# Half of w_in's remainders through ScalarE and an adding DMA, the convolution's steps dealt out anew, narrow banks added straight from PSUM

## What is computed

```
x:   4 x 4096 x 192,  weight_gen: 4 x 4096 x 8 heads x 7 taps
w    = softmax(weight_gen over the 7 taps)          (with + 1e-9 in the divisor)
conv[b,s,h,:] = sum_k w[b,s,h,k] * x[b, s-6+k, head h's 24 channels]
h    = conv @ w_in          (16384 x 192) @ (192 x 2048)
g    = h * sigmoid(1.702 h)
out  = g @ w_out            (16384 x 2048) @ (2048 x 192)
```

## Time and profile before

| | us |
|---|---|
| runs shown | 1143.32, 1144.75, 1146.94 |
| median | 1144.75 |
| the profiled execution's own time | 1144.86 |
| its span in the profile | 1143.0 |
| TensorE busy / weight loads | 1117.3 / 919.4 |
| VectorE busy | 811.0 |
| ScalarE busy | 618.5 |
| GpSimd busy | 6.5 |
| DMA | 41.89 MB, 37 GB/s on average |

### The profile page before, as it was taken

How to read it: one execution, slowest core, us unless ns; L and a number is a source line. 1 busy time by engine, 2 the same in 40 slices (tenths; PEclk the granted TensorE clock), 3 DMA queues, 4 the chain that set the end, 5 groups by cost and what they waited for, 6 DMA issues and landing times.

```text
span 1143.0 us, 21688 instructions
## 1 busy us (share of the span) xinstructions
PE 1117.3 (98%) x9748; PEld 919.4 (80%) x9748; DVE 811.0 (71%) x719; ACT 618.5 (54%) x652; POOL 6.5 (1%) x8
## 2 busy tenths in 40 slices
PE   6999979999999999999999999999999999999998
PEld 4787768888888888888888888888888888888886
DVE  7888698859587594876849578595876949678322
ACT  6466646554555645556455464645555455544543
POOL 2000000000000000000000000000000000000000
PEclk9999999999999999999999999999999999999999
DMA  7600110100101001010110101001010010100000
GB/s 243 206 15 15 52 34 20 39 29 1 39 29 39 29 1 65 2 39 29 35 33 1 39 28 40 29 1 57 11 38 29 13 55 1 39 29 1 29 1 29
DMA packets 8492, 41.89 MB, mean 37 GB/s; under 512 B 1040, under 2 KB 1296, under 8 KB 6096
## 3 DMA queue, kind: packets, MB, share of 16 engines
q1 hardware_dynamic: 8400, 40.51, 10.7%
HBM read 24.77 MB, written 12.58 MB: 33 GB/s over the span
## 4 chain that ended last, share of the span: by engine, by line
PE 91%; DVE 6%; ACT 2%; issue 1%; DMA 0%; ACTq 0%; DVEq 0%; SPq 0%
PE hid L593 43%; PE acc_main L609 28%; PE acc_rest L609 19%; DVE prod L362 1%; DVE conv L369 1%; DVE gate_lo L513 1%; ACT gate_hi L302 1%; DMA gate<-in_x_first 0%; ACT gate L299 0%; ACT xt L256 0%; DVE hid L443 0%; DVE w L415 0%; DVE xt L395 0%; DVE prod L387 0%; DVE prod L437 0%
## 5 line engine op out<-in xcount | busy, mean ns | idle before, releaser
L299 ACT ACTIVATE gate<-hid 128x1024 f32<-128x1024 f32 x256 | 263.0, 1028 | 479.6 <-PE hid L593 478.9
L513 DVE TENSOR_TENSOR gate_lo<-gate,gate_hi 128x1024 fp32r<-128x1024 f32 x256 | 312.4, 1220 | 252.2 <-ACT gate_hi L302 251.4
L593 PE MATMUL hid<-xt,w_hi 64*128 64x512 f32 x3072 | 433.6, 388 | 5.9 <-ACT xt L256 4.3
L593 PEld LDWEIGHTS hid<-xt,w_hi 64*128 64x128 f32 x3072 | 289.3, 185 | 68.6 <-issue 6.6
L609 PE MATMUL acc_main<-gate_hi,w 64*128 64x512 f32 x2048 | 317.1, 388 | 5.9 <-DVE gate_lo L513 5.9
L302 ACT ACTIVATE gate_hi<-hid 128x1024 fp32r<-128x1024 f32 x256 | 261.1, 1020 | 0.0
L609 PEld LDWEIGHTS acc_main<-gate_hi,w 64*128 64x128 f32 x2048 | 192.2, 185 | 47.5 <-DVE gate_lo L513 7.6
L593 PE MATMUL hid<-xt,w_lo 64*128 64x512 f32 x1536 | 216.8, 387 | 0.0
L609 PE MATMUL acc_main<-gate_lo,w 64*128 64x512 f32 x1024 | 200.2, 387 | 0.0
L609 PE MATMUL acc_rest<-gate_hi,w 64*128 64x512 f32 x1024 | 200.0, 387 | 0.0
L609 PE MATMUL acc_rest<-gate_lo,w 64*128 64x512 f32 x1024 | 199.9, 387 | 0.0
(11 more groups left out here) (51 smaller groups left out, 225.0 us busy)
## 6 DMA issues: line engine op xcount, KB each, us to landing
xwin<-in_x_runs SPq DMA_DIRECT2D x15, 1056.0 KB, 4.9
out<-outs_main SPq DMA_DIRECT2D x13, 512.0 KB, 2.6
out<-outs_rest SPq DMA_DIRECT2D x13, 256.0 KB, 2.9
taps<-in_tap_runs SPq DMA_DIRECT2D x1, 3136.0 KB, 10.2
taps<-in_w_rows SPq DMA_DIRECT2D x2, 1536.0 KB, 9.8
w_hi<-w_hi SPq DMA_DIRECT2D x2, 768.0 KB, 9.0
w_lo<-w_lo SPq DMA_DIRECT2D x2, 768.0 KB, 7.2
out<-outs_main SPq DMA_DIRECT2D x6, 256.0 KB, 2.0
```

The costliest lines, as they stand in the source:

```text
L299: nc.scalar.activation(gate[:, v % 2, :, :], hid[:, v % 2, :, :], ACT.Gelu_apprx_sigmoid).then_inc(gate_ready, 1)
L513: nc.vector.tensor_tensor(gate_lo[:, v % SLOTS, :, :], gate[:, v % 2, :, :], gate_hi[:, v % SLOTS, :, :], ALU.subtract).then_inc(gate_lo_r ...
L593: last = nc.tensor.matmul(hid[:, v % 2, h, :], w[rows, k if j else slice_of(h, k), q, f], xt[rows, j % 2, part, k, :], start=(i == 0), sto ...
```

## The change

Three things are changed.

1. **Remainders of w_in, columns 512 to 1,023.** VectorE's two instructions for them go. ScalarE writes -w_hi of these columns into `w_lo` (behind w_hi at the start), GpSimd issues a DMA that adds it onto `w_raw` in place (128 x 1,536 elements), and ScalarE rounds the sum into `w_lo` in two parts at n = 2 and n = 4. The rounding of w_out on ScalarE is cut in three: two parts before unit 0, the third behind unit 0.
2. **Order of the steps.** STEPS_AT has new numbers, and the steps now come from a list (STREAM) in which the four softmax steps of the piece after stand ahead of the split of the piece before. Rounding moves to v = 5 in pieces 1 and 2, and the crossings have units of their own (CROSS_HI_AT, CROSS_LO_AT). For piece 1 VectorE takes over one of the two remainder crossings.
3. **Emptying a narrow main bank.** VectorE no longer copies it into SBUF; it adds it straight from PSUM onto what ScalarE lifted, in two halves, before the `rest` half.

```diff
-STEPS_AT = ((0, 4, 2, 3, 2, 3, 3, 2),
-            (2, 2, 3, 3, 3, 3, 3, 3),
-            (1, 2, 3, 2, 3, 5, 1, 2),
-            (1, 1, 2, 2, 2, 2, 2, 4),
-            (0, 0, 0, 5, 2, 1, 2, 1, 2, 2, 1, 2, 0, 1, 0, 0))
-ROUND_AT = (7, 7, 7, 7, 12)
+STEPS_AT = ((0, 6, 2, 4, 2, 2, 2, 3),
+            (3, 3, 5, 1, 4, 5, 2, 2),
+            (0, 3, 3, 4, 2, 5, 0, 3),
+            (1, 1, 1, 1, 3, 3, 0, 4),
+            (0, 0, 1, 2, 4, 1, 2, 0, 0, 0, 3, 3, 2, 0, 1, 0))
+ROUND_AT = (7, 5, 5, 7, 12)
+CROSS_HI_AT, CROSS_LO_AT = (7, 6, 5), (7, 7, 5)
...
-            sp.wait_ge(w1_lo_ready, 5)
+            sp.wait_ge(w1_lo_ready, 3)
+            sp.wait_ge(w1_late_ready, 2)
             sp.dma_start(w1_lo[LOWER, :, 1, :].bitcast(F32), w1_lo[UPPER, :, 0, :].bitcast(F32)).then_inc(w1_doubled, 16)
...
                 act.wait_ge(xt_lo_ready, j)
-                for there, here in ((LOWER, UPPER), (UPPER, LOWER)):
+                for there, here in ((LOWER, UPPER), (UPPER, LOWER))[0:1 if j == 1 else 2]:
...
             nc.scalar.activation(w1_hi[:, :, 0, :], w1_raw, ACT.Copy).then_inc(w1_hi_ready, 1)
-            act.wait_ge(w2_loaded, 16)
-            nc.scalar.activation(w2_of(0, 2, slice(0, D)), w2_of(0, 2, slice(0, D), w2_raw), ACT.Copy
-                                 ).then_inc(w2_hi_ready, 1)
+
+            act.wait_ge(w1_hi_ready, 1)
+            nc.scalar.activation(w1_lo[:, :, 0, LATE], w1_hi[:, :, 0, LATE].bitcast(F32), ACT.Copy, scale=-1.0
+                                 ).then_inc(w1_negated, 1)
...
-            nc.scalar.activation(w2_of(2, CH // 2, slice(0, D)), w2_of(2, CH // 2, slice(0, D), w2_raw), ACT.Copy
-                                 ).then_inc(w2_hi_ready, 1)
+            act.wait_ge(w2_loaded, 16)
+            for at in (0, 2):
+                round_w2(at, at + 2)
...
+                    if n == 0:
+                        round_w2(4, CH // 2)
                     if n == 1:
                         exponentials(1)
                         exponentials(2)
+                    if n in (2, 4):
+                        at = slice((n + 2) * P, (n + 4) * P)
+                        act.wait_ge(w1_added, 16)
+                        nc.scalar.activation(w1_lo[:, :, 0, at], w1_raw[:, :, at], ACT.Copy).then_inc(w1_late_ready, 1)
...
-                        if is_narrow(j + 1):
+                    if is_narrow(j) and is_narrow(j + 1):
+                        if v == CROSS_HI_AT[j]:
                             cross_rounded(j + 1)
+                        if v == CROSS_LO_AT[j]:
                             cross_remainders(j + 1)
...
+        STREAM = [(1, q) for q in range(STEPS)] + [(2, q) for q in range(STEPS - 1)]
+        for j in range(3, LAST + 1):
+            STREAM += [(j, q) for q in range(SOFTMAX_STEPS)] + [(j - 1, STEPS - 1)]
+            STREAM += [(j, q) for q in range(SOFTMAX_STEPS, STEPS - 1)]
+        STREAM += [(LAST, STEPS - 1)]
...
+                if j == 1:
+                    dve.wait_ge(xt_lo_ready, 1)
+                    nc.vector.tensor_copy(other(j, UPPER, 1), own(j, 1)[LOWER].bitcast(F32)).then_inc(lo_crossed, 1)
...
+            def evict_main(j):
                 dve.wait_ge(main_added, UNIT0[j + 1])
+                if is_narrow(j):
+                    dve.wait_ge(main_out_act, j + 1)
+                    for to, done in ((FORE, main_summed), (AFT, main_out_dve)):
+                        of = to if j == 0 else AFT if to == FORE else FORE
+                        nc.vector.tensor_tensor(outs_main[:, 0, to], acc_main[:, 1, of], outs_main[:, 0, to], ALU.add
+                                                ).then_inc(done, 1)
+                else:
+                    wait(dve, main_stored, 16 * j)
+                    nc.vector.tensor_copy(outs_main[:, 1, :], acc_main[:, 1, :]).then_inc(main_out_dve, 1)
...
-                    if j == 0 and v in (1, 3):
-                        w1_remainder(slice((v + 3) * P, (v + 5) * P))
...
+            pool.wait_ge(w1_negated, 1)
+            pool.dma_start(w1_raw[:, :, LATE], w1_lo[:, :, 0, LATE].bitcast(F32), accum_op=ALU.add).then_inc(w1_added, 16)
...
-                    if n in (0, 1, 2, 4, 6) and i == SLICES:
-                        pe.wait_ge(w1_lo_ready, n + 1 if n < 2 else n // 2 + 2)
+                    if n in (0, 1, 2) and i == SLICES:
+                        pe.wait_ge(w1_lo_ready, n + 1)
+                    if n in (4, 6) and i == SLICES:
+                        pe.wait_ge(w1_late_ready, n // 2 - 1)
```

34 lines of the change are left out of this document (17 added, 17 removed).

## The result

| | before | after |
|---|---|---|
| median of the runs, us | 1144.79 (4 runs, 1143.32 to 1146.94) | **1128.98** (4 runs, 1128.95 to 1129.13) |
| ratio, 95% interval | | **0.9861** [0.9844, 0.9878] |
| span of the profiled execution | 1143.0 | 1127.2 |

The forecast was 1130.2, in a range of 1127.5 to 1137.5; the change is 1.2 us better than that. The kernel before scatters by more than this, and the interval of the ratio stands for a gain of 14.0 to 17.9 us, so the terms are compared in the traces, not in these times.

What follows compares the result with a forecast made beforehand. TensorE, busy for 98% of the span, was taken as the bound. Losses at the start and four piece changes fall from 19.6 to 4.9 us, so 14.7 are won: 1144.86 - 14.7 = 1130.2 us, range 1127.5 to 1137.5.

Steps and rivals of the forecast that it cites:

- Start: First units: the loss goes from 1.0 to 1.3 us, with ScalarE's added rounding and negation nearly free.
- The adding DMA: GpSimd's DMA onto w_raw at the start: lands at 26.8 us, needed at 29.1, so it costs 0.
- rival A: At the start: the adding DMA is late, landing at 33.3, costing 3.4 us and giving 1133.6; chance 0.09.
- Change 0 to 1: From piece 0 to 1: the loss falls from 4.2 to 1.3 us, 0.75 of it waiting for gate_lo(7).
- Change 1 to 2: From piece 1 to 2: the loss falls from 1.0 to 0.3 us, with gate_lo(7) due when ready.
- Change 2 to 3: From piece 2 to 3: the loss falls from 4.9 to 1.15 us, with gate_lo 0.3 and 0.5 late.
- Change 3 to 4: From piece 3 to 4: the loss falls from 8.5 to 0.85 us, with gate_lo(6) 0.5 late.
- Adding from PSUM: Narrow pieces: a copy of 0.69 us goes, the adds wait 0.6 for ScalarE's lift, so 0 is won.
- Wide pieces: Wide pieces: nothing lost; gate_lo(5) starts 6.6 us after gate(5), done at 7.8, wanted at 8.6, 0.8 in reserve.
- rival C: Wide pieces: gate_lo(5) over 0.8 us late costs each of 13 pieces; 1158.8 with the burst 3 us longer; chance 0.04.
- Rival B: Last two changes: count off by a microsecond or two, stalls over 2.5 us plus half clock, 1137; chance 0.13.
- Rival D: Whole kernel: TensorE's waits pass to another, such as the lift behind the crossings; 1144; chance 0.04.

Runs made afterwards that it cites:

- e5: Kernel after, with GpSimd waiting for gate_hi of unit 1, so the adding DMA is issued at 25.0 us: 1132.02 us.
- e6: Kernel after, with GpSimd waiting for gate_hi of unit 2, so the adding DMA is issued at 29.5 us: 1137.83 us.
- e8: Kernel after, with one step of piece 3's row moved behind the turn and no three first products in a row from piece 2 to 3: 1128.32 us.
- e9: Kernel after, with the crossings left at v = 7 at every change: 1137.03 us.
- e10: Kernel after, with the last steps of piece 4, the turn among them, moved behind the last gate_lo of piece 3: 1131.06 us.
- e2: Kernel after without the third part: the narrow main bank is copied into SBUF and added there: 1129.69 us.
- e7: Kernel after, with five wide steps in place of four in the burst at v = 4 of the wide pieces: 1144.51 us.
- e3: First and third parts alone: kernel after with the old order of steps, rounding and crossings: 1145.21 us, ratio 1.0005 to before.

## Why the prediction was right, point by point

**What bounds the kernel.** Held. Wide pieces are still 68.91 us long, 16 x 4.307, and all that was won is from the ledger.

**Start, 1.3.** Was 1.05, and TensorE has no wait there, where I had counted 0.1 and 0.2. Gate of unit 2 came at 27.15 (27.2 forecast) and the first rounding of w_lo ended at 29.8 (30.0).

**The adding DMA, 0.** Held in the kernel as it is: landing 27.5 for 26.8. It was right about the queue (engines full until w_hi's pair is through) and nearly about its work. I halved 9.0 us because the bytes are half of the pair's, which says that an adding DMA runs as fast as a copy: its bytes do move at 191 to 195 GB/s for a copy's 215 to 225. What the halving left out are the 2 us before the first bytes, which e5 and e6 show and which in the kernel after passed behind the pair. What failed is that I let each late microsecond cost one: 2.10 us of waiting cost 3.95, by the clock. So rival A's landing at 33.3 would have cost more than the 3.4 us that I gave it: e5, landed at 32.0, is 3.0 above the kernel after, where by my rule it pays 2.1. The wait that rival A rests on did not come. GpSimd's issue takes 1.42 us in the kernel after, in e5 and in e6, and in e6 the bytes move from 31.5 on, while VectorE's timeline has no gap between 28.98 and 32.88 (gate_lo, remainders of w_out, a multiplication and an addition). The Trainium skill ("SBUF — State Buffer", on SBUF's two sides) has a GpSimd DMA held behind VectorE's 2-port operations; its widest reading, that any work of VectorE holds the DMA back, falls by these rows, and its narrow one was not tried, as no float32 copy ran there. The estimate of 3.8 us worked out from the Trainium skill ("DMA: Bandwidth & Descriptors", on the anatomy of a DMA from GpSimd) does not hold for this transfer: 6.6 us is the least that was measured. Its fixed 2.0 us are near what e5 and e6 show, its 436 GB/s are not.

**Change 0 to 1, 1.3.** Was 1.04: gate_lo(7) at 48.33 for 48.8, TensorE's recorded wait 0.39 for 0.75. It costs more than is recorded: the weight loads idle 0.81 in front of it, and e5 and e6, which do not have it, are 0.68 shorter there. So 0.68 stands against 0.75 and the other 0.37 against the 0.3 that I added to each change: here the working was right.

**Change 1 to 2, 0.3.** Was 0.37, and a cause for it, which I had taken from the ledger as it stood, can now be read. Three first products stand in a row, and the third writes the `hid` that ScalarE still reads for the first. The row of 12 matmuls at 90.19 takes 1.81 where the one at 88.15 takes 1.52, and the weight loads of L630 wait 0.42 for gate_hi at 91.03, and the same 0.42 at each of the other three changes. That this is the 0.37 was not tried by itself: at the change 2 to 3, e8 does without the three in a row, and a wait of 0.44 for another buffer comes in its place.

**Change 2 to 3, 1.15: the term that was mis-sized.** Was 0.41. I had gate_lo(6) late by 0.3 and the first one of piece 3 by 0.5. VectorE's timeline at units 5 and 6, and the weight load that wants gate_lo(6):

```profile
108.72 1.22 DVE L548 TENSOR_TENSOR gate_lo<-gate,gate_hi 128x1024 fp32r<-128x1024 f32 x1
...
115.68 1.22 DVE L548 TENSOR_TENSOR gate_lo<-gate,gate_hi 128x1024 fp32r<-128x1024 f32 x1 [0.41 <-ACT gate_hi L313]
...
116.96 0.30 PEld L646 LDWEIGHTS acc_main<-gate_hi,w 64*128 64x128 f32 x4 [0.18 <-DVE gate_lo L548]
```

Gate of unit 5 starts at 106.37, so VectorE comes to gate_lo(5) 2.35 behind it and not 2.8. The steps behind that took about what I gave them, the split ends 5.57 behind gate(5) for 6.15, and gate_lo(6) 10.53 for 11.1; it is wanted at 10.6 to 10.7, so it costs next to nothing (the 0.41 is the 0.37 of the change before and 0.04). VectorE even waits for ScalarE there (0.41, and 0.61 at gate_lo(7)), and the first gate_lo of piece 3 ends at 127.64, 0.45 ahead of the product that wants it (128.09), where I had it 0.5 late. The step that was mis-sized is thus the time at which VectorE reaches gate_lo(5), 0.45 too late in my count; that is most of the first of the two terms and half of what the second was off by, and the other half is not traced. The order depends on the crossings far more than I said: e9 puts 8 us on their places.

**Change 3 to 4, 0.85.** Was 1.03: 0.33 of recorded waiting for gate_lo, 0.76 at the weight loads, which is worth 0.6 (0.5 forecast), and 0.4 that stays, as at the other changes. Moving one step behind the turn takes the 0.6 away (e8), moving the turn behind the last gate_lo adds 1.9 (e10).

**Adding from PSUM, 0.** Was worth 0.5, once, at the change 2 to 3 (e2). I had set the copy saved against the wait for ScalarE's lift and reckoned only with the bank; the eviction also stands ahead of the first gate_lo of the new piece.

**Wide pieces, 0, and rival C.** Held: gate(5) 521.23, gate_lo(5) 527.80, 6.57 later, 6.6 forecast. The rival was right in kind: e7 pays in each of 13 pieces. Its turning point was too far off, since the reserve is 0.6 and not 0.8: the gain is gone with 1.7 us more in the burst, where by my count it took 1.9 (0.8 of reserve and 14.7 / 13).

**Rival B** (a microsecond or two, and then the half clock) did not come about. e9 shows the pattern that it describes, idle 4.53 and then a clock of 0.50, but at one change and not at the last two; that it took 1137.03 where I gave 1137 is a coincidence. **Rival D** did not come about; e3 is its picture, where work taken off VectorE turns into a wait.

**The sum.** The five terms were off by 0.25, 0.26, -0.07, 0.74 and -0.18 us, 1.0 of the 1.2 by which the time was missed. The marks at v = 3 came at 62.93, 97.75, 132.61 and 168.09 for 63.3, 98.1, 133.7 and 169.0.

**The x window of piece 2,** the shortest cover in the change: issued at 47.42, landed 8.8 later at 56.2, used at 58.20. 2 us of it were left.

What stays open: the 1.05 us of the start have not been traced to a wait, and no run takes away the three first products in a row without bringing in another wait.

## What to carry to other kernels

Where one engine is busy for 98% of the span, make a ledger: the pace of the steady part times its units, and the marks of one instruction that recurs, a whole period apart. It says where each microsecond is lost, and it names the term of a forecast that failed.

On an engine that works in order, move what others wait for (the turn, a crossing that frees a buffer) ahead of what has slack, and count the slack at each place from its own row: here work taken off VectorE was worth 0.6 us, and the same steps in another order 14. A wait costs more than its length where the clock falls behind it, so take the longest ones first.

## What the runs showed of the hardware that was not expected

- **An adding DMA within SBUF** (float32, 786 KB, 400 packets) moves 191 to 195 GB/s with the engines to itself, and takes 6.6 to 7.0 us, of which some 2 us pass before the first bytes. Copies within SBUF without an addition move 215 to 225 GB/s in the kernel after (36 to 42 us), and loads from HBM and stores there reach 410 GB/s from 50 to 55 us. So both kinds of transfer within SBUF run at about half the rate of the loads.
- **The clock behind a wait.** It was 0.50 from 34 to 36 us in e5, behind 2.10 us of waiting, and 1.00 in every window from 156 to 172 us in e10, behind waits of 1.54 and 0.38. A wait of 6.92 us in e6 cost 9.69.
- **Scatter.** The kernel before spreads over 3.6 us, e3_old_order over 2.2, e5_add_later over 2.1 and e9_cross_at_7 over 1.3; the kernel after over 0.18 and the others over 0.8 or less. The four that scatter all have waits of over 2 us at which the clock falls; e6_add_too_late has one too and spreads over 0.7 only, so why they scatter stays open. Where they do, the longer executions have the lower mean clock (the kernel before: 0.997 to 0.998 up to 1143.4 us, 0.995 to 0.996 above).
